# The order in which TensorE reads the routing logits' moving operand: feature run inside, or token group inside

## The reference

```python
# stage A: for each of 8 x 8 heads, 576 positions, 64 dims, 32 memory slots
a = softmax(phi); k_m = a.T @ k; v_m = a.T @ v
attn = softmax(q @ k_m.T / 8); attn_out = attn @ v_m
x = attn_out.transpose(0, 2, 1, 3).reshape(4608, 512)
# stage B: a gated feed-forward layer, and after it the routing
h = x @ w_in                      # 512 -> 2048
x2 = (h * sigmoid(1.702 * h)) @ w_out
logits = x2 @ w_gate              # 512 -> 8 experts
e_idx = argmax(logits, axis=1)    # one expert for each token
eom = sigmoid(x2 @ w_output_gate) # 512 -> 8
# stage C: each token goes through its one expert, scaled by its gates
ye = relu(x2[mask] @ w1[e]) @ w2[e]
out[mask] = gate_w[mask, None] * eom[mask, e, None] * ye
```

## Time and profile before

| | before |
|---|---|
| median of three runs | 1364.31 us |
| profiled execution, its own time | 1364.31 us |
| its span on the core | 1362.6 us |
| TensorE matmul busy | 1321.4 us (97%) |
| VectorE busy | 655.3 us (48%) |
| ScalarE busy | 390.7 us (29%) |
| GpSimd busy | 523.6 us (38%) |
| mean granted TensorE clock | 0.996 of full |

### The profile page before, as it was taken

The page is one execution under the profiler, slowest core; times in us unless marked ns, Lnnn a source line. Parts: engine busy times, 40 slices in busy tenths (PEclk is TensorE's granted clock), DMA queues, the critical chain, the costliest instruction groups (busy, mean ns, idle before and its releaser), DMA issues.

```text
span 1362.6 us, 25709 instructions
## 1 busy us (share of the span) xinstructions
PE 1321.4 (97%) x7778; PEld 1075.6 (79%) x7779; DVE 655.3 (48%) x1352; ACT 390.7 (29%) x725; POOL 523.6 (38%) x623
## 2 busy tenths in 40 slices
PE   6888999999999999999999999999999999999997
PEld 4565888888888888888888888887788888888885
DVE  5898233353433533434334344347555555555552
ACT  3455222232222222322223222223322222222221
POOL 2202783353354433434434334511433242433341
PEclk9999999999999999999999999999999999999998
DMA  9997446657576465464654646557873789549871
GB/s 329 372 395 270 130 148 181 193 192 195 192 203 200 161 187 193 163 176 168 185 192 164 177 175 186 165 172 253 234 224 100 220 236 256 160 139 264 243 229 57
DMA packets 155931, 275.29 MB, mean 202 GB/s; under 512 B 17380, under 2 KB 54549, under 8 KB 153829
## 3 DMA queue, kind: packets, MB, share of 16 engines
q1 hardware_dynamic: 98804, 205.35, 45.2%
q10 hardware_dynamic: 43600, 37.37, 11.3%
q0 software_dynamic: 13472, 31.88, 7.6%
HBM read 146.03 MB, written 100.45 MB: 181 GB/s over the span
## 4 chain that ended last, share of the span: by engine, by line
PE 94%; DVE 2%; ACT 1%; DMA 1%; issue 1%; ACTq 0%; SPq 0%; POOL 0%; DVEq 0%; POOLq 0%
PE ps L660 29%; PE ps L694 29%; PE ps L735 16%; PE ps L764 15%; PE ps L622 2%; PE ps L609 1%; PE ps L594 1%; PE ps L637 1%; DMA phT<-in_phi 1%; PE ps L704 1%; DMA kvm<-in_kv 1%; PE ps L629 0%; ACT xo L876 0%; ACT kk L859 0%; ACT kmT L868 0%
## 5 line engine op out<-in xcount | busy, mean ns | idle before, releaser
L660 PE MATMUL ps<-xs,W 128*128 (+1 forms) x1728 | 417.6, 390 | 1.4 <-DVE xs L1153 1.4
L694 PE MATMUL ps<-W,gs 128*128 128x512 f32 x1728 | 415.0, 389 | 0.1
L660 PEld LDWEIGHTS ps<-xs,W 128*128 128x128 f32 x1728 | 322.8, 188 | 71.1 <-issue 2.7
L694 PEld LDWEIGHTS ps<-W,gs 128*128 128x128 f32 x1728 | 324.3, 188 | 67.8 <-DVE gs L1203 0.5
L1201 DVE TENSOR_TENSOR gate<-ps,gate 128x512 f32<-128x512 f32 x144 | 99.5, 691 | 363.4 <-ACT gate L927 363.2
L764 PE MATMUL ps<-W,chT 128*128 (+1 forms) x936 | 218.4, 389 | 0.9 <-DVE chT L1338 0.9
L927 ACT ACTIVATE gate<-ps 128x512 f32<-128x512 f32 x144 | 86.1, 598 | 464.3 <-PE ps L660 463.8
L735 PE MATMUL ps<-W,cx 128*128 (+1 forms) x936 | 218.5, 389 | 0.8 <-issue 0.8
L1538 POOL CAST whi<-raw 128x512 fp32r<-128x512 f32 x128 | 83.9, 656 | 323.6 <-DMA raw<-in_moe_w 323.5
L764 PEld LDWEIGHTS ps<-W,chT 128*128 128x128 f32 x936 | 175.5, 188 | 38.3 <-issue 2.0
L735 PEld LDWEIGHTS ps<-W,cx 128*128 128x128 f32 x936 | 175.6, 188 | 37.7 <-issue 1.4
(11 more groups left out here) (158 smaller groups left out, 805.0 us busy)
## 6 DMA issues: line engine op xcount, KB each, us to landing
W<-expert_scratch SPq DMA_DIRECT2D x24, 2048.0 KB, 11.0
raw<-in_moe_w SPq DMA_DIRECT2D x128, 256.0 KB, 2.8
expert_scratch<-whi SPq DMA_DIRECT2D x128, 256.0 KB, 2.8
expert_scratch<-raw SPq DMA_DIRECT2D x128, 256.0 KB, 3.0
cq<-ch ACTq DMA_DIRECT2D x156, 128.0 KB, 4.1
kvm<-in_kv SPq DMA_DIRECT2D x16, 1152.0 KB, 7.9
crec<-record_scratch POOLq DMA_DIRECT2D x160, 64.0 KB, 3.6
qT<-in_q SPq DMA_DIRECT2D x16, 576.0 KB, 6.9
```

Of the source, the lines that this page charges most:

```text
L660: mm = pe.matmul(ps[:, f % 2, :], W[:, col:col + P], xs[:, bass.ds(x0 + (x_lo * K1 + c) * T, T)], start=(c == 0 and w_lo + x_lo == 0), sto ...
L694: mm = pe.matmul(ps[:, 2 + s, :], gs[:, f % 2, g_lo, s * P:(s + 1) * P], W[:, col:col + DM], start=(f == 0 and g_lo + w_lo == 0), stop=(f ...
```

## The change

In `moved`, the two innermost dimensions of the moving operand change places. Before, the innermost run is eight neighbouring float32 values (`n`), and the plane `h` is outside it. After, the plane is innermost (four values that lie 2048 bytes apart), and `n` is outside it. The set of elements that a matmul reads, and their number (128 for each partition), stay the same; their order, and so the order of the output's columns, changes. The columns come out in the order of the tokens, so `moved_columns` goes, and VectorE's transpose L1235 reads PSUM in one contiguous row of 128. The last tile (`copied`) is as before. On every engine the instructions, their number and their order are the same.

```diff
--- before.py
+++ after.py
@@ -708,7 +708,7 @@
             def moved(c, a):
 
 
-                return x2x[:, 0:4, :].rearrange("p h (s c n) -> p c s h n", s=SUB, c=K1)[:, c, :, :, 8 * a:8 * a + 8]
+                return x2x[:, 0:4, :].rearrange("p h (s c n) -> p c s n h", s=SUB, c=K1)[:, c, :, 8 * a:8 * a + 8, :]
 
             def copied(c, a):
 
@@ -1228,11 +1228,11 @@
                         (hold if then_wait == "hold" else wait)(dve, s, done[0])
                 return step
 
-            def route1(t, by_token):
+            def route1(t):
 
                 wait(dve, b_lg, t + 1)
                 step = steps_of(b_rt, RT * t)
-                step(dve.transpose(lg[:].rearrange("p s e -> p (s e)"), by_token(ps[:, 7, 0:P])), "hold")
+                step(dve.transpose(lg[:].rearrange("p s e -> p (s e)"), ps[:, 7, 0:P]), "hold")
                 dve.max(mx8[:, 0, :], lg[:, 0, 0:NE]).then_inc(b_lfree, 1)
                 for s in range(1, SUB):
                     step(dve.max(mx8[:, s, :], lg[:, s, 0:NE]), "hold" if s == SUB - 1 else False)
@@ -1249,10 +1249,6 @@
                 step(dve.tensor_reduce(og[:], osel[:], AX.X, ALU.add), False)
                 step(dve.tensor_copy(base[:, 0, :], base[:, SUB, :]))
 
-            def moved_columns(lgT):
-
-                return lgT.rearrange("p (s h n) -> p s n h", s=SUB, h=4)
-
             def route2(t):
 
                 wait(dve, b_cnt, t + 1)
@@ -1349,7 +1345,7 @@
                         if 4 <= f < 4 + SUB:
                             x2_t(t - 1, f - 4)
                         if f == 9:
-                            route1(t - 1, moved_columns)
+                            route1(t - 1)
                         if f == 12:
                             route2(t - 1)
                     if not last and 11 <= f < 11 + K1:
@@ -1369,7 +1365,7 @@
                 dve.tensor_copy(xraw[:, s, :], ps[:, LAST_BANK[s], :]).then_inc(b_x2Tv, 1)
             dve_relu(0, 0)
             dve_x_lo(2, 0)
-            route1(NT - 1, lambda lgT: lgT)
+            route1(NT - 1)
             route2(NT - 1)
             ends()
             dve_h_t(0, 0)
```

## The result

The changed kernel takes 1370.7 us, the median of five runs (1369.38 to 1373.02), and the kernel before 1364.31 us (1361.72 to 1366.88). The ratio is 1.0058, with a 95% interval of 1.0038 to 1.0078: slower by 6.4 us, with the whole interval above 1.

A forecast was written before the change was run, and what follows sets the result against it. The prediction took TensorE's gapless row of matmuls in stage B as the bound. To 1364.3 us it added 0 for VectorE's transpose and 6.8 for TensorE's single-element reads, giving 1371.1 us, with an 8-in-10 range of 1363.4 to 1388.

The forecast's parts named there:

- the piece that was to grow from 1.01 to about 1.9 us: Stage B, L704's part of the chain of waits around one tile's logits: expected to lengthen in the first eight tiles.
- What bounds the kernel: Stage B: TensorE is busy 706.00 of 706.00 us, so any lengthening of its matmuls reaches the end one for one.
- VectorE's transpose, term 0: L1235 reading PSUM in a row gains nothing: it stays at 0.3 us, with 5.8 us of cover.
- The cover of what waits for the logits: The next load_x has 7.4 us to spare before its first reader, so longer logits cause no further wait.
- TensorE's read: L704's moving operand, eight tiles: single-element reads add 0.108 us to a round of four strips, 6.8 us taken in all.
- what a record pays: One L704 matmul: 128 single elements at ScalarE's stepped price of 0.91 ns add 0.116 us.
- a round of four strips as bound by one strip's columns: L704: 128 columns need about 0.118 us of a 0.126 us round, leaving 0.008 us of slack.
- the four strips pay it side by side: L704: the 0.116 us comes once for each round of four strips, not once for each record.
- Rival B: L704's strips pay one after another, wholly (1394 us) or from a half (1379), middle 1382; chance 0.20.
- Rival C: TensorE's moving reads in L704 absorb the jumps, a single-element read taking under 0.98 ns; 1364.3 us, not slower; chance 0.31.

## Why the prediction was right, and where it was so by luck

The forecast was 1371.1 us; the median is 1370.7, and the piece that was to grow from 1.01 to about 1.9 us grew to 1.86. The records grew from 273 to 393 ns, just over the 370 to 390 foretold.

What bounds the kernel: right, and shown. TensorE's row has no gap in stage B, and a longer block arrives at the end as it is; the kernels with the logits four times over show it: 20.9 us of time for 21.0 of added pieces, and 29.8 between the two patterns for 27.9.

VectorE's transpose, term 0: right, and shown alone. The order has no effect on this reader, 0.30 to 0.32 us either way; the note of the Trainium skill that the prediction weighed here ("SBUF — State Buffer", "Door 1: The DMA port swizzle") speaks of matmuls.

The cover of what waits for the logits: right. The load lands 8.8 us ahead of its reader.

TensorE's read, +0.85 us for a tile, 6.8 in all: the sum came out, three of its steps did not. I took 0.116 us for what a record pays, from ScalarE's stepped writes, and a record alone pays 0.064. I took a round of four strips as bound by one strip's columns, with 0.008 us of slack, from the durations of records in rows 7; the kernel with one strip after another shows 0.075 us for a record, so a round has 0.051 us over what one strip needs. The durations of pipelined records, even their differences, did not give the pace. With the right two numbers, and strips that pay side by side, the sum would have been 0.8 us, within the noise. The missing 6 us come from the step "the four strips pay it side by side": they do so only in part. Four strips with single elements need 0.2325 us a round and not the 0.138 of one, as four strips with runs of eight need 0.126 and not 0.075. With the measured overlap of 2.4 the 2.04 us of the strips alone come to the 0.85 us of the changed kernel. Rival B had the mechanism, in part, but with a price by which even half of it came to 1379. That the errors cancelled was not to be seen in advance.

Rival C had an argument that the runs decide: a float32 column was thought to leave 0.92 ns for an element. It leaves 0.48 (7.93 us for 32 x 512 columns), little more than the 0.44 of the fast matmuls. By its own condition C needed a single-element read under 0.98 ns; alone it takes 16.77 us for 32 x 512, 1.02 ns, and 4.43 us for 32 x 128, 1.08 ns.

What stays open: what the strips share. The dependence on their distance points to a clash of addresses in the memory, and no run here shows more than that. Nor do the runs explain the full-array matmuls, where steps of 2 and pairs are as dear as steps of 4 while four far elements in turn cost little. With single elements in four planes, distances of the strips beyond the three measured were not tried. No pattern in these runs was faster than runs of eight, so no version that beats the kernel before came of it.

## What to carry to other kernels

Where TensorE is the bound, keep neighbours in the innermost run of the moving operand. In the float32 strips runs of four cost nothing (1.01 us) and pairs a tenth (1.09 to 1.12); in the full array runs of four still cost 3.20 us in place of 2.72. Give the permutation to a reader that has time and doesn't pay for it, as VectorE's PSUM transpose does in the kernel before. To price an access on TensorE, take the distance between starts of the same records in a row, with and without neighbours beside them; neither the record's duration nor another engine's price for a stepped access is a substitute.

## What the runs showed of the hardware that was not expected

- Four 32-column strips together are not four times one strip: 1.01 us against 2.39 with runs, 1.86 against 4.43 with single elements, 2.4 times as fast in both; two strips together are almost twice as fast (1.26 and 2.40).
- The relative place of the strips' operands changes a block of the same size from 1.86 to 2.5 and 2.7 us.
- In full-array matmuls of 512 columns (0.227 us in a row), steps of 2 and of 4 elements cost the same, 0.46 us, pairs in different planes 0.45, fours 0.27, and single elements in four planes in turn only 0.28.
